# Gathering the first expert of the second MoE layer before the last rows are routed

## The reference

```python
def _moe_ref(x, w_skip, w_gate, w1, w2):            # layer 1: N=1536 rows, D=512, E=8, F=1024
    do_compute = x @ w_skip > 0
    out = x.copy()
    xc = x[do_compute]
    logits = xc @ w_gate
    e_idx = np.argmax(logits, axis=1)
    ...                                             # gate_w: softmax value of the chosen expert
    for e in range(E):
        mask = e_idx == e
        h = np.maximum(xc[mask] @ w1[e], 0.0)
        y[mask] = gate_w[mask, None] * (h @ w2[e])
    out[do_compute] = xc + y
    return out

def _moe2_ref(x, w_gate, w1, w2, capacity):         # layer 2: capacity 384
    logits = x @ w_gate
    expert_idx = np.argmax(logits, axis=1)
    ...                                             # gate_w as above
    for i in range(N):                              # in row order: the first `capacity` rows of an expert
        e = expert_idx[i]
        if counts[e] < capacity:
            disp[e, counts[e]] = x[i]; pos[i] = counts[e]; counts[e] += 1; keep[i] = True
    h = np.maximum(np.einsum('ecd,edf->ecf', disp, w1), 0.0)
    y = np.einsum('ecf,efd->ecd', h, w2)
    out[i] = gate_w[i] * y[expert_idx[i], pos[i]]   # for rows kept, else 0
```

## Time and profile before

| | us |
|---|---|
| median of 3 timed runs | 402.98 (401.69 to 403.48) |
| the profiled execution | 401.76, span 400.0 |
| attention and routing of layer 1 | to 80.9 |
| layer 1, eight jobs of 13.1 | 80.9 to 187.2 |
| between the layers | 187.2 to 200.9 |
| layer 2, eight jobs of 23.3 | 200.9 to 389.6 |
| last scaling, scatter, end | 389.6 to 400.0 |

### The profile page before, as it was taken

The page is one execution under the profiler, slowest core; times in us unless marked ns, Lnnn a source line. Parts: engine busy times, 40 slices in busy tenths (PEclk is TensorE's granted clock), DMA queues, the critical chain, the costliest instruction groups (busy, mean ns, idle before and its releaser), DMA issues.

```text
span 400.0 us, 7602 instructions
## 1 busy us (share of the span) xinstructions
PE 383.2 (96%) x2857; PEld 344.3 (86%) x2857; DVE 260.6 (65%) x462; ACT 171.3 (43%) x217; POOL 82.7 (21%) x79
## 2 busy tenths in 40 slices
PE   7999998999999999999899999999999999999990
PEld 5888887789899988998688998989989898998980
DVE  2876877859989888976496567463654736365420
ACT  2354443514433443251354445455544545554410
POOL 4010000321543323231600330403003040300100
PEclk9999999999999999999999999999999999999997
DMA  7999997399999999539299967766737676610100
GB/s 254 361 378 382 355 346 257 99 338 397 390 389 390 386 385 364 185 109 341 77 369 377 379 225 252 225 219 222 263 133 270 209 235 188 226 65 0 52 26 8
DMA packets 56243, 101.22 MB, mean 253 GB/s; under 512 B 6662, under 2 KB 18822, under 8 KB 56081
## 3 DMA queue, kind: packets, MB, share of 16 engines
q1 hardware_dynamic: 46432, 85.87, 60.4%
q0 software_dynamic: 4416, 11.18, 8.2%
q10 hardware_dynamic: 5360, 3.70, 2.9%
HBM read 89.58 MB, written 12.73 MB: 256 GB/s over the span
## 4 chain that ended last, share of the span: by engine, by line
PE 87%; DMA 5%; DVE 2%; issue 2%; ACT 1%; POOL 0%; SPq 0%; DVEq 0%; ACTq 0%; POOLq 0%
PE ps_h L1352 36%; PE ps_y L1378 27%; PE ps_s L1194 3%; PE ps_u L1206 3%; PE ps_r L1240 3%; PE ps_o L1227 3%; PE ps_y L1394 3%; PE ps_t L1323 2%; PE ps_o L1219 2%; DMA fits<-flags,slot_row 2%; DMA flags<-fits 2%; PE ps_h L1181 1%; DMA table<-in_consts 1%; DMA xg<-x_rows,slot_in 1%; PE ps_t L1415 0%
## 5 line engine op out<-in xcount | busy, mean ns | idle before, releaser
L1001 DVE TENSOR_TENSOR w_lo<-raw,w_hi 128x2048 fp32r<-128x2048 f32 x48 | 109.1, 2288 | 23.2 <-ACT w_hi L701 20.4
L701 ACT CAST w_hi<-raw 128x2048 fp32r<-128x2048 f32 x48 | 90.4, 1905 | 4.3 <-PE ps_y L1378 3.0
L1012 DVE SCALAR_TENSOR_TENSOR h_lo<-ps_h,h_hi 128x512 fp32r<-128x512 f32 x48 | 33.0, 690 | 60.9 <-ACT h_hi L710 60.9
L1378 PE MATMUL ps_y<-w_hi,h_hi 128*128 128x512 f32 x176 | 70.9, 403 | 0.0
L710 ACT ACTIVATE h_hi<-ps_h 128x512 fp32r<-128x512 f32 x48 | 28.7, 597 | 94.6 <-PE ps_h L1352 94.6
L1378 PE MATMUL ps_y<-w_hi,h_lo 128*128 128x512 f32 x176 | 68.8, 391 | 0.0
L1378 PE MATMUL ps_y<-w_lo,h_hi 128*128 128x512 f32 x176 | 68.7, 391 | 0.0
L1352 PEld LDWEIGHTS ps_h<-x_f,raw 128*128 128x128 f32 x512 | 58.4, 192 | 1.3 <-issue 0.7
L1352 PE MATMUL ps_h<-x_f,raw 128*128 128x128 f32 x512 | 58.7, 276 | 0.3 <-ACT x_f L706 0.3
L1352 PE MATMUL ps_h<-x_hi,w_hi 128*128 128x256 f32 x256 | 41.4, 284 | 0.3 <-ACT x_hi L706 0.2
L1352 PE MATMUL ps_h<-x_lo,w_hi 128*128 128x256 f32 x256 | 41.3, 284 | 0.0
(11 more groups left out here) (163 smaller groups left out, 429.6 us busy)
## 6 DMA issues: line engine op xcount, KB each, us to landing
raw<-in_moe_w SPq DMA_DIRECT2D x64, 1024.0 KB, 7.7
q_t<-in_q_cols SPq DMA_DIRECT2D x16, 192.0 KB, 6.7
k_t<-in_k_cols SPq DMA_DIRECT2D x16, 192.0 KB, 6.7
x_rows<-rows ACTq DMA_DIRECT2D x8, 384.0 KB, 6.0
k_in<-in_k_rows SPq DMA_DIRECT2D x15, 192.0 KB, 6.8
v_in<-in_v_rows SPq DMA_DIRECT2D x15, 192.0 KB, 6.8
out<-zero SPq DMA_DIRECT2D x1, 2816.0 KB, 21.2
w_wide<-w_next SPq DMA_DIRECT2D x1, 2048.0 KB, 14.3
```

The source lines that it names most:

```text
L701: nc.scalar.copy(w_hi[c], raw[:, 4 * job.par + c, :]).then_inc(hi_done[c], 1)
L1001: nc.vector.tensor_tensor(w_lo[c], raw[:, 4 * job.par + c, :], w_hi[c].bitcast(F32), ALU.subtract).then_inc(lo_done[c], 1)
L1012: nc.vector.scalar_tensor_tensor(out=h_lo[:, cols], in0=ps_h[:, g % 2, :], scalar=0.0, in1=h_hi[:, cols].bitcast(F32), op0=ALU.max, op1=AL ...
L1378: last = pe.matmul(ps_y[:, t, :], ht, wt, start=(fb == 0 and z == 0), stop=(fb == 2 * QB - 1 and z == 2))
```

## The change

For job 0 of layer 2 alone:

- The map is read before the last chunk (G+1, the slots of job 7) is in it. DVE's `find_first` makes 2 x 128 row numbers; a slot that isn't filled yet gets row N of `x`, which holds zeros. POOL's `gather_first` gathers them after the scatters of jobs 0 to 6 have landed and ahead of the scatter of job 7, and signals `first_in`.
- The rows of job 7 that belong to this expert are added on PE: four products of `yo` with the fp32 one-hot `late_hot` start the sums in `ps_t`, and the transposes of the gathered rows (`turn_first`) are accumulated on them. ACT copies the result in two halves (`copy_first`).
- In group 0 of job 0's `hidden` the three passes run over both blocks in turn, the pass with `x_lo` last.
- At the end of each window of layer 2, PE clears `ps_t` by two products of zeros, and DVE and POOL do `find_first` and `gather_first` for the window that would follow; POOL raises `window_stored` after that.

And around it: `cross_counts` and the making of `fits` move from layer 2's first `step` to the end of layer 1 (into `ps_y[:, 1]`), and the store of the flags follows the first relu of layer 2. In layer 1's step of job 6, DVE does `add_y` first, `choose_next` ahead of relu 0, and splits, relu 1 and `place` in another order; on PE `next_counts` and `late_logits(0)` stand in the middle of `hidden(7,1)` and `late_counts(0)` after two blocks of `output(7,2)`. `keep_clock(11)` and the hold `first_sent` go. `win.read` moves behind six jobs. SP's holds name the new signals. The semaphores `ident_in` and `cap_in` are merged into others.

```diff
@@ SP
                         if first and a == 1:
-                            sp.wait_ge(gathered[1][0], 32)
+                            hold(sp, first_in, n_win * 32)
...
-                    sp.wait_ge(turned[1], 1)
+                    sp.wait_ge(gathered[1][1], 32)
@@ POOL
+                def gather_first():
+                    for t in range(2):
+                        nc.gpsimd.indirect_dma_start(
+                            out=xg[:, 0, t], out_offset=None, in_=x,
+                            in_offset=bass.IndirectOffsetOnAxis(ap=first_id[:, t:t + 1], axis=0),
+                            bounds_check=N, oob_is_err=False).then_inc(first_in, 16)
...
-                    for e in range(ahead):
+                    for e in range(i, ahead):
                         gather(Job(layer, base, w, e // 2, e % 2))
-                        if i == 1 and e == 0:
-                            nc.gpsimd.memset(sent[:], 0.0).then_inc(first_sent, 1)
...
+                    if i == 0:
+                        for a in range(2):
+                            hold(pool, yo_free[0][a], (w * (E // 2) + E // 2 + 1 - a) * 16)
+                        hold(pool, first_ids, w + 1)
+                        gather_first()
                     scatter(Job(layer, base, w, E // 2 - 1, 1), by_block=i == 1)
                     for a in range(2):
                         hold(pool, yo_free[i][a], (w * (E // 2) + E // 2 + 1) * 16 * tb)
+                    if i == 0:
+                        hold(pool, first_in, w * 32 + 32)
+                    else:
+                        hold(pool, first_ids, n_first + w + 1)
+                        gather_first()
+                        hold(pool, first_in, (n_first + w + 1) * 32)
                     pool.sem_inc(window_stored[i], 1)
@@ ACT, layer 2's first job
-                        act.wait_ge(ids_ready[1], w + 1)
+                        copy_first(first)
+                        split(first, 2)
+                        relu(first, 0)
+                        hold(act, fits_ready, first_fits)
+                        act.dma_start(flags.rearrange("(p g) e -> p g e", g=G), fits[:, 0:G]).then_inc(flags_stored, 16)
                         nc.scalar.activation(ex[:], below[:], ACT.Exp).then_inc(exp_done[1], 1)
@@ DVE, step of job 6 in layer 1
+                        add_y(this)
                         split(nxt, 2)
-                        add_y(this)
-                        split(nxt, 3)
-                        relu(nxt, 0)
                         dve.wait_ge(lg2_in, w * 16 + 16)
                         choose_next(wchain)
-                        relu(nxt, 1)
+                        relu(nxt, 0)
...
                         ranks_next(wchain)
-                        place(1, range(G)).then_inc(slots_ready[1], 1)
+                        split(nxt, 3)
                         dve.wait_ge(late_done, w * LATE + 1)
                         dve.wait_ge(next_free[this.par], this.half * 16 + 16)
                         choose_late(0, wchain)
+                        relu(nxt, 1)
+                        place(1, range(G)).then_inc(slots_ready[1], 1)
+                        dve.wait_ge(hot_ready[1], w * 3 + 2)
+                        carry_next(G, G + 1)
+                        dve.wait_ge(rank_done[1], w * 3 + 2)
+                        rank_late(0, wchain)
+                        place(1, [G]).then_inc(slots_ready[1], 1)
@@ DVE, end of layer 1
+                        dve.wait_ge(first_mapped, w + 1)
+                        find_first(wchain)
...
+                        nc.vector.tensor_scalar(late_hot[:], iota_b[:], rank1[:, G + 1:G + 2], late_first[:, 0:1], ALU.is_equal, ALU.mult
+                                                ).then_inc(late_placed, 1)
+                        place(1, [G + 1]).then_inc(slots_ready[1], 1)
+                        dve.wait_ge(crossed, w + 1)
+                        find_fits(wchain)
@@ DVE, start and end of layer 2's window
+                    if i == 1:
+                        split(first, 0)
...
-                        dve.wait_ge(first_sent, w + 1)
-                        split(first, 0)
                         split_x(first)
                         split(first, 1)
+                        relu(first, 0)
...
+                        hold(dve, first_mapped, first_maps + w + 1)
+                        find_first(wchain)
@@ PE, end of layer 1
-                        pe.wait_ge(slots_ready[1], w * 3 + 1)
+                        pe.wait_ge(slots_ready[1], w * 3 + 2)
                         map_next(range(G))
+                        map_next([G]).then_inc(first_mapped, 1)
                         turn_y(1)
                         late_logits(1)
...
+                        pe.wait_ge(above_ready, w + 1)
+                        cross_counts()
+                        pe.wait_ge(late_placed, w + 1)
+                        for kk in range(KD):
+                            pe.matmul(ps_t[:, kk * 2 * P:(kk + 1) * 2 * P], yo[:, 1, kk * P:(kk + 1) * P], late_hot[:],
+                                      start=kk % 2 == 0, stop=False, skip_group_check=True)
                         pe.wait_ge(slots_ready[1], w * 3 + 3)
                         map_next([G + 1]).then_inc(slots_mapped[1], 1)
```

More of the change, by code:

```diff
@@ L39 @@
 PRE = 2 * P
-CROSS = PRE + P
 class Layer:
@@ L330, in __init__ @@
                 self.turn = w * (E * layer.tb // 4) + (2 * pair + a) // (4 // layer.tb)
+                if layer.i == 1 and a % 2 == 0:
+                    self.turn = w * (E // 2 - 1) + (2 * pair + a) // 2 - 1
             def rows_of(self, t):
@@ L773, in _ @@
                         split(first, 3)
[L774 to L778, removed]
+                        copy_x(first)
+                        relu(first, 0)
+                        relu(first, 1)
+                    for g in range(2, layer.groups):
                         relu(first, g)
+                    later_jobs(act, layer, base, w, step)
                     win.read(w)
-                    later_jobs(act, layer, base, w, step)
                     last_two = last_jobs(layer, base, w)
@@ L1325, in turn, with turn_first, hidden @@
                     last.then_inc(turned[i], 1)
-                def hidden(job, c):
-                    if c == 0:
+                def turn_first(job):
+                    hold(pe, first_in, (n_first + w) * 32)
+                    for kk in range(KD):
+                        for t in range(tb):
+                            last = pe.matmul(ps_t[:, kk * cap + t * P:kk * cap + (t + 1) * P], job.rows_of(t)[:, kk * P:(kk + 1) * P], ident,
+                                             start=False, stop=True, is_transpose=True, skip_group_check=True)
+                        if kk == 1:
+                            last.then_inc(first_half, 1)
+                    last.then_inc(turned[1], 1)
+                def hidden(job, c, part=range(layer.fpg), first=False):
+                    if c == 0 and part[0] == 0:
                         pe.wait_ge(x_hi_done[i], job.n + 1)
@@ L1340, in hidden @@
                             pe.wait_ge(h_lo_done[i], job.n * layer.groups + g - 1)
-                        for fl in range(layer.fpg):
+                        if i == 0:
+                            terms = [(raw[:, 4 * job.par + c, :], x_f)]
+                        else:
+                            terms = [(w_hi[c], x_hi), (w_lo[c], x_hi), (w_hi[c], x_lo)]
+                        order = [(fl, z) for fl in part for z in range(len(terms))]
+                        if first and g == 0:
+                            order = [(fl, z) for z in range(len(terms)) for fl in part]
@@ L1354, in hidden @@
-                        last_of_chunk = g == (c + 1) * (i + 1) - 1
-                        last.then_inc(chunk_used[c] if last_of_chunk else h_done, 1)
+                            wt, xt = terms[z]
+                            if z == 2 and c == 0 and g == 0 and fl == 0:
+                                pe.wait_ge(x_lo_done[i], job.n + 1)
+                            for kk in range(KD):
+                                last = pe.matmul(dst, wt[:, kk * QF + fb * P:kk * QF + (fb + 1) * P], xt[:, kk, :],
+                                                 start=(kk == 0 and z == 0 and not (first and g == 0 and fl > 0)),
+                                                 stop=(kk == KD - 1 and z == len(terms) - 1), skip_group_check=True)
@@ L1357, in wait_output @@
+                        if part[-1] == layer.fpg - 1:
+                            last_of_chunk = g == (c + 1) * (i + 1) - 1
+                            last.then_inc(chunk_used[c] if last_of_chunk else h_done, 1)
                 def wait_output(job, c, fb):
```

139 lines of the change are left out of this document (73 added, 66 removed).

## The result

The changed kernel takes 403.67 us (median of 11 runs) against 401.69 for the kernel before (11 runs, 400.84 to 403.66) timed beside it: a ratio of 1.0053 [1.0033 to 1.0073], 2.0 us slower, where +0.1 was forecast. One of the 11 runs took 2136 us, for a reason that nothing here shows; the other ten lie between 402.34 and 406.80, their median is 403.60, and the ratio is made without the long one. The profiled run took 403.0, its span 401.2.

A forecast was written before the change was run, and what follows sets the result against it. TensorE was busy 383.2 of 400.0 us, so only its gaps and critical waits could be gained. -5.9 up to the steady jobs and +6.0 at the end gave +0.1 on 402.98: 403.1 us, range 400.5 to 406.0.

The forecast's parts named there:

- Layer 1's last jobs: Reordered step of job 6 on DVE and PE: PE stalls 0.2 to 0.3 before late_counts(0), output(7) ends later, +0.2 us.
- rival C: End of layer 1: PE's stall is a whole split (2.3) instead of 0.3, giving 405.1 to 405.5; chance 0.05.
- The first gather: Between the layers: ids at 188.85 instead of 192.75, second transfer landing 5.9 us later as before, at 194.75.
- Rival B: Between the layers: first gather lands late, PE waits in turn_first; 405.6, or 408.8 at the longest; chance 0.14.
- The last rows beside it: Job 7's routing and one-hot products (1.8 us) end at 194.1, 0.65 before the gather, which ends last.
- my upper bound: Late one-hot products between the layers twice as slow: +1.8 us, of which 1.15 would show.
- D: Between the layers: routing plus one-hot products end last, so the path isn't shortened; 404.3 at twice the price, no separate chance.
- Start of layer 2: hidden(0) starts at 196.75, output(0) at 208.35 instead of 213.70 (-5.35); map_final no longer waits (-0.5).
- POOL's queue: Splits lock out indirect DMA issues; gather_first isn't hit, job 1's gather is held but covered by 5 us.
- The end: After the final scatter: gather for a next window that doesn't come, not hidden, +6.0 us (bounds +5.7 to +6.7).
- the side that had 0.19: Slower outcomes, rivals B and C together, beyond 2 us of 402.98: chance 0.19.
- The forecast's last line: Sign of failure: the prediction is wrong if the drain shrinks, or if turn_first or turn(1) waits.

The follow-up runs named there:

- after: The full changed kernel, first profile, against the kernel before: 403.67 us, ratio 1.0053.
- e1: Changed kernel without the gather for a next window behind the last scatter of layer 2: 397.54 us, ratio to the kernel before 0.9871.
- e2: Changed kernel with one more keep_clock call before late_counts(1) and one after the crossing counts: 403.61 us, ratio 1.0027.
- e6: Changed kernel with the end gather's ids made between the halves of the last output and the gather issued ahead of the last scatter: 399.11 us, ratio 0.9943.
- e8: e1 with e12's extra keep_clock calls, the map ahead of layer 1's last six matmuls and find_first ahead of add_y: 397.03 us, ratio 0.9892.
- e10: e1 again, unchanged, in a second batch on the same chip as the changed kernel: 398.91 us, ratio to the kernel before 0.9912.
- e12: e1 with the two extra keep_clock calls of e2: 398.05 us, ratio 0.9895.
- e3: e2 with the scatter of job 7 held until the first gather has landed: 404.19 us, ratio 1.0020.
- e9: e8 without the two extra keep_clock calls: 398.07 us, ratio 0.9888.
- e5: e1 with crossing counts, making of fits and store of the flags put back in layer 2's first step: 397.55 us, ratio 0.9933.
- e4: Changed kernel with the end gather's bound set to N - 1, so that it moves no data: 401.78 us, ratio 0.9973.
- after again: The changed kernel unchanged, run for a second profile in another batch: 405.36 us, ratio to the kernel before 1.0073.

## Why the forecast's range held and its value was low

**Layer 1's last jobs: right.** +0.2 forecast, +0.14 measured. DVE was at `choose_late(0)` at 181.4 and PE waited 0.27 in front of `late_counts(0)`, the 0.2 to 0.3 of the replay; rival C (a stall of a whole split) is refuted.

**The first gather: mechanism right, price too low.** The ids came at 188.17, where 188.85 was expected; 0.47 of that is the earlier start of the whole stretch. The step that failed is "same two transfers, same quiet DMA: lands 5.9 after the ids". In its new place the second transfer took 4.97 (after), 4.4 (e1), 4.3, 5.40, 4.4, 3.78, 5.96 (e2 to e6), 4.3 (e8) and, by the start of the transposes, 4.3, 5.0 and 5.0 (e10 to e12), 4.7 in the mean, against 3.70 and 4.03 in the old one. I had taken one row, 3.70, though the median of all such landings was 4.4; with that the term is 0.7 smaller. (That median is of both layers; the 16 transfers of layer 2 alone have 4.2, and 7.8 as the longest. The 9.4 is one of layer 1.) Rival B was therefore half true: not a lost case of 0.14, but a shift of the middle by 1.0 us, and up to 2.3 in one execution (e6). The cause of the spread is open. The scatter is excluded by e3, the weight loads of SP by the traces. At the end, where all 256 slots read row N, the landings of after, e2, e3 and e6 took 3.8 to 4.3, so those reads alone don't make 5 or 6; ACT's and DVE's work beside it wasn't tried apart. The forecast's last line called itself wrong if `turn_first` waits: it waited 0.27 in after and 0.37 again, which its own sum allowed (0.65), and up to 2.83 in e6, which it didn't.

**The last rows beside it.** 1.8 us was forecast for the one-hot products and 3.56 measured, at half clock; the crossing products ended at 191.5, before 192.2 as forecast. That is my upper bound, but for a reason that I didn't have. The nearness of the two ends (D) was right: 195.2 and 195.35 in after, and in e1, e8 and e9 the products end last. I had let the clock stay up without asking. That the loss of `keep_clock(11)` is the reason isn't shown: in the kernel before it stood behind this stretch, at 192.5, and the clock stayed up there in both profiles.

**Start of layer 2: right.** `hidden(0)` to `output(0)` took 11.63 (11.6 forecast), and `output(0)` to `output(1)` 24.14 instead of 24.98, -0.84 where -0.5 was forecast. The crossing counts and the flags alone are 1.4 in this stretch (e5), of which 0.5 is left over the whole transition.

**POOL's queue: right.** The two issues of `gather_first` took 1.04 and 1.02. Beside a split an issue is again long and ends 0.87 and 0.89 behind it, in after (timeline):

```profile
193.03 3.07 POOL L564 DMA_INDIRECT next_rows<-next_lg,slot_row  x1 [0.30 <-issue]
...
198.60 2.97 POOL L535 DMA_INDIRECT xg<-x_rows,slot_in  x1 [0.31 <-issue]
```

The second is job 1's gather; PE didn't wait for it at `turn(1)`, nor in e3, where it was issued only at about 205.4.

**The end: mechanism right, price 0.7 too low.** From the last scatter's landing to the first issue 1.04 (1.0 forecast), to the second 1.35 (1.35), to the release 4.3 (3.7; the bound was 4.4), and the drain 0.16 longer. Again the one row of 3.70 was the wrong one.

**The sum.** +0.14 -3.15 -2.0 +6.7 = +1.7, against +2.0 of 401.69 in the timed runs; with the stall of DVE +2.7, against +3.3 in the batch whose profiles show it (405.36 against 402.01). There the account isn't complete: the profiled execution, stall included, took 403.02 and is the fastest of the ten. The forecast of 403.1 against the earlier median of 402.98 was +0.1. That 403.67 lies so near to 403.1 is partly luck: the kernel before measured 401.69 in more runs, 1.3 less than the median of three from which I counted. The range held also as a difference in this batch (+2.0, where it reached to +3.0), and not in the second (+3.3). What came is 2.0 us, at the edge of what a measurement of this kernel can tell, and on the side that had 0.19. One row, 3.70, stood in two terms, and I let them cancel. In the sum they don't cancel: a longer landing makes the gain smaller and the cost greater, so its error counts twice.

## What to carry to other kernels

Preparation for a next turn of a loop is paid in the last turn too, and there nothing hides it: here two indirect DMAs of nothing cost 4.6 us, and with data 6.7, more than the early gather gains. Issue it before the last visible work ends (e6: 3.7 us back) or leave it out of the last turn. When a gather is taken off the path, price its landing by the median of its kind, not by the row of one lucky execution, and allow for the clock of the engine that waits for it (1.6 us in e6, nothing in e3).

## What the runs showed of the hardware

- TensorE's clock fell to half (0.50) in a stretch where it ran small matmuls, idle for 0.22 us at most, in three profiles (after, after again, e1) and not in three others with the same code there (e4, e6, e10); products of 1.9 to 2.0 us then took 3.5 to 3.7. After 2.83 us idle it was low for the first 3.4 us of new work (e6); after 2.07 us idle it was not (e3).
- POOL's final drain has a length of its own: 5.46 us in the eight profiles without the end gather, 5.63 in the six with it, also where that gather moves nothing (e4) or stands before the last scatter (e6).
- An indirect DMA that moves nothing lands 2.1 us after its issue; one of 256 KB in the two places of `gather_first` lands after 3.3 to 6.0.
- On one chip DVE stood 3.0 us in front of one instruction for which the trace shows nothing to wait for, in three of four profiles there, and cost `hidden(0)` 1.0 to 1.7 us.
